# A chain of row counts inside the loop of halves, and later scale pieces, in a routed MLP kernel on one core

## The reference

```
attention: 8 heads of 64; heads 0-3 see 32 keys back, heads 4-7 every 4th of 128 keys back
x = attention output, one row per token
e_idx  = argmax(x @ w_gate)                       # one of 8 experts per token
gate_w = softmax(x @ w_gate)[e_idx]; eom = sigmoid(x @ w_output_gate)[e_idx]
y      = gate_w * eom * (relu(x @ w1[e_idx]) @ w2[e_idx])     # w1 512x1024, w2 1024x512
out    = softplus(y @ w_in) @ w_out               # w_in 512x2048, w_out 2048x512
```

## Time and profile before

| | |
|---|---|
| median of 3 executions | 843.73 us (842.26 to 846.15) |
| profiled execution | 846.15 us, its span 844.4 us |
| PE busy | 775.8 us (92%) |
| DVE, ACT, POOL busy | 52%, 47%, 26% |
| mean granted clock of PE | 0.959 of full |

### The profile page before, as it was taken

How to read it: one execution, slowest core, us unless ns; L and a number is a source line. 1 busy time by engine, 2 the same in 40 slices (tenths; PEclk the granted TensorE clock), 3 DMA queues, 4 the chain that set the end, 5 groups by cost and what they waited for, 6 DMA issues and landing times.

```text
span 844.4 us, 14065 instructions
## 1 busy us (share of the span) xinstructions
PE 775.8 (92%) x4658; PEld 699.0 (83%) x4659; DVE 440.5 (52%) x905; ACT 399.3 (47%) x1014; POOL 222.1 (26%) x218
## 2 busy tenths in 40 slices
PE   5999994786879999899979999999999999999996
PEld 3667674586879999889979999989999999999995
DVE  8885987754444567676555334343334334334332
ACT  3885983133343556455454344335334335335332
POOL 6220220742264366578570000001001001001001
PEclk9999997598889999899999999999999999999999
DMA  9577202454253546566430000000000000000000
GB/s 250 164 188 269 93 0 112 134 177 146 83 181 121 167 165 220 184 184 203 166 100 2 1 13 25 0 0 38 0 0 37 0 0 37 0 0 38 0 0 37
DMA packets 27262, 74.62 MB, mean 88 GB/s; under 512 B 4112, under 2 KB 12320, under 8 KB 26720
## 3 DMA queue, kind: packets, MB, share of 16 engines
q1 hardware_dynamic: 20624, 53.52, 19.7%
q0 software_dynamic: 5744, 16.02, 6.2%
q10 hardware_dynamic: 864, 4.72, 1.4%
HBM read 64.79 MB, written 9.45 MB: 88 GB/s over the span
## 4 chain that ended last, share of the span: by engine, by line
PE 86%; DVE 6%; issue 4%; ACT 2%; DMA 1%; SPq 1%; POOL 0%; DVEq 0%; ACTq 0%
PE bank L614 13%; PE bank L616 12%; PE bank L615 12%; PE bank L638 8%; PE bank L640 8%; PE bank L636 8%; PE bank L494 4%; PE bank L627 4%; PE bank L629 4%; PE bank L628 4%; PE bank L518 2%; PE bank L531 2%; PE bank L504 2%; DVE w_lo L1071 1%; DMA v_sb<-vw 1%
## 5 line engine op out<-in xcount | busy, mean ns | idle before, releaser
L1183 DVE SCALAR_TENSOR_TENSOR g_sb<-bank,soft 128x384 f32<-128x384 f32 x96 | 53.5, 558 | 234.8 <-ACT soft L881 234.8
L877 ACT ACTIVATE soft<-bank 128x384 f32<-128x384 f32 x96 | 47.2, 492 | 208.7 <-PE bank L616 208.7
L614 PE MATMUL bank<-x_parts,w_hi 128*128 (+1 forms) x352 | 115.4, 328 | 22.6 <-issue 18.7
L1071 DVE TENSOR_TENSOR w_lo<-raw,w_hi 128x1024 fp32r<-128x1024 f32 x68 | 90.1, 1326 | 68.2 <-ACT w_hi L813 68.2
L466 POOL DMA_INDIRECT out<-y_sb,out_rows_i x18 | 17.5, 970 | 378.7 <-ACT y_sb L888 375.1
L616 PE MATMUL bank<-x_parts,w_lo 128*128 (+1 forms) x352 | 114.3, 325 | 0.0
L615 PE MATMUL bank<-x_parts,w_hi 128*128 (+1 forms) x352 | 114.1, 324 | 0.0
L813 ACT ACTIVATE w_hi<-raw 128x1024 fp32r<-128x1024 f32 x68 | 71.7, 1058 | 59.6 <-PE bank L629 58.8
L614 PEld LDWEIGHTS bank<-x_parts,w_hi 128*128 128x128 f32 x352 | 70.3, 200 | 25.8 <-issue 24.7
L627 PE MATMUL bank<-h_hi,w_hi 128*128 128x384 f32 (+3 forms) x256 | 81.3, 317 | 4.2 <-DVE h_lo L1089 4.2
L750 ACT ACTIVATE probs<-bank,neg_max 96x128 f32<-96x128 f32 x192 | 67.3, 365 | 23.5 <-DVE neg_max L920 23.4
(11 more groups left out here) (197 smaller groups left out, 1805.1 us busy)
## 6 DMA issues: line engine op xcount, KB each, us to landing
raw<-we SPq DMA_DIRECT2D x64, 512.0 KB, 3.3
x_tokens<-x_sb ACTq DMA_DIRECT2D x6, 768.0 KB, 5.1
v_sb<-vw SPq DMA_DIRECT2D x4, 1024.0 KB, 13.2
raw_m<-wm POOLq DMA_DIRECT2D x8, 512.0 KB, 5.1
raw<-wm SPq DMA_DIRECT2D x8, 512.0 KB, 3.3
q_sb<-qT SPq DMA_DIRECT2D x4, 768.0 KB, 8.6
k_sb<-kT SPq DMA_DIRECT2D x8, 384.0 KB, 11.5
v_sb<-vw SPq DMA_DIRECT2D x4, 512.0 KB, 4.7
```

The source lines that it names most:

```text
L614: nc.tensor.matmul(bank_[:, 0:rows], hi[:, w], x_part(0, k), start=(k == 0), stop=False)
L1071: nc.vector.tensor_tensor(w_lo[:, r, :], raw[:, r, :], w_hi[:, r, :].bitcast(F32), ALU.subtract).then_inc(w_lo_done, 1)
```

## The change

Four edits in one diff. On PE, the tree of branches becomes a chain: size 384 is tested first, then 352, and so on, and the loop over the two halves is now outside it, so the chain is walked once per half and every copy stands inside the one loop. `scale_ps` moves from the second half of bank 3, which it shared with `source_ps`, to bank 4. On DVE, the five operations that split the scales into pieces move behind the writing of the row numbers. And the four clears `zero_y` move from before the wait for the summed scales to behind `scale_first(0)`; `scale_first(1)` and `scale_first(2)` are placed among and behind the operations that find the row counts. (Bank 4 is one of the banks that `zero_y` clears.)

```diff
-        rank_ps, tot_ps, source_ps, scale_ps = bank[1], bank[2], bank[3][:, 0:P], bank[3][:, P:2 * P]
+        rank_ps, tot_ps, source_ps, scale_ps = bank[1], bank[2], bank[3], bank[4]
...
-                def of_size(sizes):
-                    if len(sizes) == 1:
-                        with pe.Fori(0, HALF) as half:
-                            half_slot_products(slot, half, parity, sizes[0])
+                def from_size(half, n):
+                    if n == len(SIZES) - 1:
+                        half_slot_products(slot, half, parity, SIZES[n])
                         return
-                    middle = len(sizes) // 2
-                    with pe.If(taken > sizes[middle]):
-                        of_size(sizes[:middle])
-                    with pe.If(taken <= sizes[middle]):
-                        of_size(sizes[middle:])
-
-                of_size(SIZES)
+                    with pe.If(taken > SIZES[n + 1]):
+                        half_slot_products(slot, half, parity, SIZES[n])
+                    with pe.If(taken <= SIZES[n + 1]):
+                        from_size(half, n + 1)
+
+                with pe.Fori(0, HALF) as half:
+                    from_size(half, 0)
...
             step(V.reciprocal(R["scale"][:, :], R["den"][:, :]))
-            step(V.tensor_copy(scale_piece[:, 0, :], R["scale"][:, :]))
-            (the four other operations on scale_piece)
             dve.wait_ge(sources_summed, 1)
...
             V.tensor_scalar(half_source_i[:, 1, :], source[:, :], 2.0, 1.0, ALU.mult, ALU.add
                             ).then_inc(half_sources_ready, 1)
+            step(V.tensor_copy(scale_piece[:, 0, :], R["scale"][:, :]))
+            (the four other operations on scale_piece)
             V.tensor_tensor(block_scale[:, :, :, :],
...
-            for k in range(KC):
-                zero_y(k)
             dve.wait_ge(scales_summed, 1)
...
             dve.wait_ge(row_scales_ready, 1)
+            scale_first(0)
+            for k in range(KC):
+                zero_y(k)
             step(V.tensor_tensor(slot_cmp[:, :, :], SL["expert8"][:, :].unsqueeze(2).to_broadcast([P, SLOTS, E]),
                                  over_slots(emin8[:, :]), ALU.is_equal))
             step(V.tensor_tensor(X["end"][:, :], count, X["row"][:, :], ALU.add))
             step(V.tensor_tensor(slot_tmp[:, :, :], slot_cmp[:, :, :], over_slots(X["end"][:, :]), ALU.mult))
+            scale_first(1)
...
             V.tensor_copy(taken_i[:, :], SL["taken"][0:1, :]).then_inc(sizes_ready, 1)
-            for j in range(TPS):
-                scale_first(j)
+            scale_first(2)
             split_lo(0, 1)
```

More of the change, by code:

```diff
@@ L1062, in _ @@
                             ).then_inc(half_sources_ready, 1)
+            step(V.tensor_copy(scale_piece[:, 0, :], R["scale"][:, :]))
+            step(V.tensor_tensor(R["rest"][:, :], R["scale"][:, :], scale_piece[:, 0, :], ALU.subtract))
+            step(V.tensor_copy(scale_piece[:, 1, :], R["rest"][:, :]))
+            step(V.tensor_tensor(R["rest"][:, :], R["rest"][:, :], scale_piece[:, 1, :], ALU.subtract))
+            step(V.tensor_copy(scale_piece[:, 2, :], R["rest"][:, :]))
             V.tensor_tensor(block_scale[:, :, :, :],
```

## The result

| | before | after |
|---|---|---|
| median | 843.86 us (842.26 to 846.15, 4 runs) | 854.15 us (852.86 to 854.78, 4 runs) |
| ratio to before | | 1.0118, 95% interval 1.0092 to 1.0145 |
| profiled execution, its span | 846.15 us, 844.4 us | 856.93 us, 855.2 us |

The account below looks back on a forecast made before the run. PE-bound (TensorE busy 92% of the span), so only its gaps and waits matter. Terms +2.4 + 3.0 - 2.2 + 0.5 + 3.6 + 1.8 = +9.1 us on the median 843.73 gave 852.8 us; range 844.0 to 861 (forecast's own 848.5 to 858).

Parts of the forecast that it names:

- scale path: DVE ahead of the slots: moved piece operations and clears make h_lo late, +1.8 us; bounds 1.0 and 2.7.
- levels at slot starts 4, 5, 6: Two more unchosen branch tests, 0.4 us each, before the 288- and 224-row slots, with no slack: together +2.4 us.
- levels in the middles: Between halves of slots 4, 5 and 6, the second walk outlasts the sequencer's lead: PE idle, +3.0 us.
- code fetches: Slots 0 to 2: stalls on code not at hand move, -2.2 us, plus 0.5 for the 288 body's second part.
- clock: PE in the slots: one and a half more clock falls behind new gaps, 2.4 us each, +3.6; bounds 0 and +7.2.
- (a): Middle of slot 0: first jump to the chain's end stalls 4.2 us, of which PE sees 2.1.
- (c): Middle of slot 1: the jump to the chain's end misses again, 5.0 us.
- (b): Before slot 1, into the 288 alternative: one stall instead of two, gap falling from 10.15 to about 5.1 us.
- (1): Rival: the chain's end stays fetched, so no stall or clock fall in slot 1's middle; +1.7, 845.4 us; chance 0.20.
- (2): Rival: clock falls at every new gap, five more falls, and the start costs 2.7; +18.4, 862 us; chance 0.13.
- (3): Rival: spreading fetches hides them, only the 288 alternative still misses; -4.1, 839.6 us; chance 0.08.
- (4): Rival: code held only near the running block, every walk fetches; +29 or more, over 870 us; chance 0.04.

Follow-up runs that it names:

- PE half alone: Kernel before with only the branch edit: chain of sizes inside the loop of halves, DVE as before; 852.9 us, ratio 1.0133.
- the kernel with the loop in each alternative: Kernel before with the tree made a chain, walked once per slot; 852.16 us, ratio 1.0115; on the second chip 865.19 us, ratio 1.008.
- reversed chain: Kernel before with a six-size chain inside the loop of halves, testing 224 rows first and 384 last, DVE as before; 859.51 us, ratio 0.9987.
- with four: Unused sizes 352 and 256 left out: of the kernel before, 849.55 us, ratio 0.9876; of the kernel after, 848.7 us, ratio 0.9889 against the kernel before.
- DVE half alone: Kernel before with scale path, clears and scale_ps as in the kernel after, the tree as before; 846.06 us, ratio 1.0036.

## Why the prediction was right, step by step

| term | forecast | profile after |
|---|---|---|
| scale path, at the first product of line 627 | +1.8 | +1.5 |
| levels at slot starts 4, 5, 6 | +2.4 | gaps 2.06, 2.83, 2.17: +2.7 |
| levels in the middles | +3.0 | 0.44, 1.48, 1.47: +3.4 |
| code fetches, with 0.5 for late code | -1.7 | 2.43, 3.69, 5.13, 0.65 for 10.15, 5.29: -3.5 |
| clock | +3.6 | some +5.4 |
| breaks in the stream of products | none | some +1.3 |
| sum | +9.1 | +10.8 of span; +10.3 in the medians |

Every term that the prediction summed is there. That 9.1 came so near to 10.3 is in part luck: fetches and scale path came out 2.1 us lower, levels, clock and a cost that it did not have 3.8 us higher. The column is one pair of profiles, both a little over their medians (2.3 and 2.8 us).

- **Levels.** Right within 0.1 us at each place named: 1.96, 2.74, 2.10 were forecast and 2.06, 2.83, 2.17 found. With the equal gaps of the PE half alone and their absence from the middles of the kernel with the loop in each alternative, shown. A level that is not chosen has a price as soon as the sequencer's lead is used up.
- **Fetches.** Three slow branches where they were put. (a) 2.1 forecast, 2.43 found. (c) 5.0 and 5.13. (b) was mis-sized: 5.1 forecast, 3.69 found, as this branch took 3.0 us instead of 4 to 6. The trace fits a fetch that was already under way (a packet of queue 8 comes 0.6 us behind the branch's start, at 208.5 us, where it comes 2.0 and 2.4 us behind at the other two), but no run here isolates that. The gap (d) before slot 2 was 0.65, not 1.0. That code first reached from slot 0 has to be fetched again in slot 1 is seen in every kernel with six sizes except the reversed chain, and in none with four; what takes its place is not shown.
- **The clock** is the step that was mis-sized most: +3.6 forecast, some +5.4 found. Number and price were both off, in opposite directions. The prediction counted one and a half more falls at 2.4 us; there were four more, and most lasted 3.4 us, so cost 1.7. Its own rows give 27.0 - 24.4 = 2.6 us for a fall of 6.8 us, not 2.4. All edge gaps (2.43, 2.06, 2.17) led to a fall in this profile, and one of 1.80 us. Another execution has others: the PE half alone, with the same gaps, had five falls, and none at its gaps of 2.05, 2.15 and 1.80 us.
- **The scale path** was right at line 627 and wrong on the way. The first product comes 3.3 us later, not 2.5. Two things went wrong there. The last scale_first ends 3.3 us later instead of 2.7 (162.51 + 0.8 for 159.98): beside the moved operations, line 1128 takes 0.61 us instead of 0.17 and the three scalings 1.54 us instead of 1.26. And the prediction took ACT's start as the bound and credited the transposes of tiles 0 and 1 that go ahead. They do (ACT starts 0.6 us behind the last scale_first instead of 1.5), but the bound is PE's sequencer, which starts its reads only behind the third tile and needs 2.9 us from there; this credit is worth nothing at the first product. The wait for h_lo, 1.20 in place of 2.60, gave more back than expected.
- **What else moved.** The listed gaps of the slots grew by 2.5 us, -1.4 at h_lo makes the +1.1 of idle PE. The parts sum to 1.5 + 2.5 + 6.8 = 10.8 us of span, the 6.8 being the pace from the first product of line 627 to the last MLP. In it 5.4 us are clock, and 1.3 of the other 1.4 are the five new breaks, a term that the prediction did not have.
- **The rivals.** (1), the end of the chain stays fetched, is wrong with six sizes (5.13 us in the middle of slot 1) and right with four (0.22 us). (2) was half right: four more falls instead of five, each cheaper, none behind the middles of 1.48 and 1.47 us, and the start cost 1.5 and not 2.7. (3) is excluded by three slow branches. (4), code held only near the running block, is excluded: the window of two blocks that the Trainium skill states (Runtime: NRT & Kernel Launch, Instruction fetch mechanics) would have made later jumps stall, and none of 85 does. The same section gives PE, unlike other engines, room for 2048 instructions; six bodies of some 240 would fit in that, and yet code is fetched twice here, so neither figure alone describes these traces. What the page says of a stall behind a taken branch to code not at hand does fit: 3.0 to 4.7 us each.

## What to carry to other kernels

In this kernel a branch is free only as long as the engine's sequencer is ahead of the engine, and in a loop it must be paid per turn: read the sequencer's lead at the end of a body, and compare it with the levels walked there. Copies of a program that no input uses aren't free either: taking two of six out was worth 1.2%, more than any reordering of the branches. When a busy TensorE gets short gaps, add the clock: cost every new gap of about 2 us or more with a fall, and every break in the stream of products with some 0.25 us, and compare kernels by their medians, as single profiles differ in the number of falls.

## What was not expected of the hardware

- A jump over up to five copies costs PE's sequencer only 0.2 us once all is fetched; in the kernel after there was no packet of queue 8 between 249.5 and 442 us (the other instruction queue, 14, had one, at 374 us).
- Stalls on code ranged from 3005 to 6407 ns (the longest in the DVE half alone), the same places giving nearly the same number in different kernels (4399, 4219 and 4339; 3005 and 3005).
- In the slots PE stood at 0.50 for 3.4 or 6.8 us at a time and, with a long gap in it, for 10.2 or 13.7 us. Of the 22 gaps of 1.94 to 2.83 us at starts of slots without a slow branch, over all profiles, 18 had a fall at them; those of 1.15 to 1.5 us mostly had none, but three of 1.30 to 1.33 us did.
- The profile named a semaphore of DVE for the wait ahead of slot 0, and the bound was PE's sequencer, which reads two counts into registers there (492 and 327 ns for the two loads, 2.9 us with all that stands around them).
- Two chips differ by some 15 to 17 us in the same kernel, 13 of them in one wait at the end of the slots (5.34 and 18.32 us); the cause is open.
- A change in PE's code of the slots went with a late start of the attention part, 150 us earlier in time, on both chips (3.27 and 1.58 us of wait for v_sb instead of 0.5 and 0.37, and 6.8 us of PE at 0.50 beside it). The wait alone doesn't make the start late: the kernel after waits 1.3 us for v_sb and starts line 578 0.8 us earlier than before. No run here explains it.
